# Loading the first expert's weights in two blocks and zero-filling the output rows during attention

## What is computed

```python
x = attention(q, k, v)                    # 2 batches x 768 tokens x 512, 8 heads of 64
# window |i-j| < 16, beside 24 block summaries (max of k, mean of v, blocks of 32)
e = argmax(x @ w_gate)                    # or the previous token's expert, by a local gate
p = softmax(x @ w_gate)[e]
x = p * (relu(x @ w1[e]) @ w2[e])         # 8 experts, 512 -> 1024 -> 512
theta = x @ w_theta
u = x + w_tok_r @ (x * cos(theta)) + w_tok_i @ (x * sin(theta))
out = u + relu(u @ w_ch)
```

## Time and profile before

| what | value |
|---|---|
| median of 3 runs | 424.57 us |
| lowest and highest of them | 423.96 and 425.23 us |
| the profiled execution's own time | 423.96 us |
| its span, first to last instruction | 422.2 us |
| mean granted clock of TensorE | 0.999 |
| PE busy | 409.2 us, 97% |
| DVE, ACT and POOL busy | 258.0, 194.1 and 80.8 us |
| moved by DMA | 54.50 MB, mean 129 GB/s |

### The profile page before, as it was taken

One profiled execution on the slowest core, in us unless ns is written; L12 is line 12 of the kernel. 1 busy time (PEld: TensorE's weight loads), 2 busy tenths in 40 slices (PEclk: granted clock), 3 DMA queues, 4 the chain that ended last, 5 costly groups with the idle time before them and its releaser, 6 DMA issues.

```text
span 422.2 us, 8097 instructions
## 1 busy us (share of the span) xinstructions
PE 409.2 (97%) x2791; PEld 328.6 (78%) x2792; DVE 258.0 (61%) x429; ACT 194.1 (46%) x431; POOL 80.8 (19%) x127
## 2 busy tenths in 40 slices
PE   6889999999999999999999999999999999999996
PEld 3668786468888888888888778888888888888885
DVE  4898998898646327363117595666687646454352
ACT  1698995624647326463247464444433143213110
POOL 3697783221112100121110023200000000000000
PEclk9999999999999999999999999999999999999999
DMA  8995551162989933518130025300000000000012
GB/s 293 412 374 170 185 178 78 51 249 73 380 274 397 367 153 90 208 35 338 50 100 26 0 72 202 100 2 0 0 2 0 26 25 0 27 25 27 25 57 93
DMA packets 17424, 54.50 MB, mean 129 GB/s; under 512 B 2033, under 2 KB 2161, under 8 KB 17137
## 3 DMA queue, kind: packets, MB, share of 16 engines
q1 hardware_dynamic: 12560, 40.98, 27.1%
q0 software_dynamic: 2960, 9.70, 7.0%
q10 hardware_dynamic: 1872, 3.41, 2.1%
HBM read 40.46 MB, written 13.63 MB: 128 GB/s over the span
## 4 chain that ended last, share of the span: by engine, by line
PE 77%; DVE 3%; ACT 3%; DVEq 1%; issue 1%; ACTq 0%; POOL 0%
PE ps L1570 15%; PE ps L1572 14%; PE ps L1571 14%; PE ps L1714 8%; PE ps L1715 8%; PE ps L1716 8%; PE ps L1652 2%; PE ps L1592 2%; PE ps L1621 2%; PE ps L1460 2%; ACT w_h L756 1%; PE ps L1565 1%; DVE w_l L1095 1%; PE ps L1432 1%; DVEq L1102 1%
## 5 line engine op out<-in xcount | busy, mean ns | idle before, releaser
L1714 PE MATMUL ps<-z_h,mix_h 128*128 128x512 f32 x144 | 56.9, 395 | 0.0
L1716 PE MATMUL ps<-z_h,mix_l 128*128 128x512 f32 x144 | 56.1, 390 | 0.0
L1715 PE MATMUL ps<-z_l,mix_h 128*128 128x512 f32 x144 | 56.1, 390 | 0.0
L1570 PE MATMUL ps<-w_h,hT_h 128*128 128x512 f32 x104 | 42.0, 404 | 0.8 <-DVE w_l L1095 0.5
L1095 DVE TENSOR_TENSOR w_l<-w_raw,w_h (+1 forms) x32 | 37.4, 1219 | 8.3 <-ACT w_h L756 8.3
L705 ACT ACTIVATE p<-s,nmax 128x120 f32<-128x120 f32 x96 | 36.5, 384 | 11.1 <-DVE nmax L938 11.1
L1572 PE MATMUL ps<-w_l,hT_h 128*128 128x512 f32 x104 | 40.7, 391 | 0.0
L1571 PE MATMUL ps<-w_h,hT_l 128*128 128x512 f32 x104 | 40.5, 390 | 0.0
L1570 PE MATMUL ps<-w_h,xT_h 128*128 128x512 f32 x96 | 38.4, 400 | 0.0
L1571 PE MATMUL ps<-w_h,xT_l 128*128 128x512 f32 x96 | 37.4, 390 | 0.0
L1572 PE MATMUL ps<-w_l,xT_h 128*128 128x512 f32 x96 | 37.4, 390 | 0.0
(11 more groups left out here) (264 smaller groups left out, 860.2 us busy)
## 6 DMA issues: line engine op xcount, KB each, us to landing
w_raw<-w SPq DMA_DIRECT2D x32, 512.0 KB, 6.2
mix_raw<-mix SPq DMA_DIRECT2D x6, 768.0 KB, 6.0
kfull<-k_full SPq DMA_DIRECT2D x8, 400.0 KB, 6.4
q_all<-q_t SPq DMA_DIRECT2D x6, 512.0 KB, 7.3
vpad<-v_pad SPq DMA_DIRECT2D x4, 768.0 KB, 8.8
xd<-x_sb POOLq DMA_DIRECT2D x12, 256.0 KB, 4.6
ys<-y_sb ACTq DMA_DIRECT2D x12, 256.0 KB, 2.0
out<-o SPq DMA_DIRECT2D x12, 256.0 KB, 2.0
```

The source lines that it names most:

```text
L1570: pe.matmul(ps[:, bank, :], a_h[:, k, :], w_h[:, n, :], start=(k == 0), stop=False)
L1714: pe.matmul(ps[:, i, :], w_h, zh, start=(jb == 0 and m == 0), stop=False)
L1715: pe.matmul(ps[:, i, :], w_h, zl, start=False, stop=False)
L1716: mm = pe.matmul(ps[:, i, :], w_l, zh, start=False, stop=(jb == TPB - 1 and m == 1))
```

## The change

Three edits, two on SP and one on ACT.

```diff
             sp.dma_start(const[:, C_UT:C_END], const_d[:, C_UT:C_END]).then_inc(rconst_in, 16)
-            for i in range(STEPS):
-                sp.wait_ge(norm_done, 2 + i)
-                sp.dma_start(w1_raw[:, i * SW:(i + 1) * SW, :], w1_d[0, :, i * SW:(i + 1) * SW, :]).then_inc(w1_in[i], 16)
-            for i in range(STEPS):
-                sp.wait_ge(norm_done, 2 + STEPS + i)
-                sp.dma_start(w2_raw[:, i * SW:(i + 1) * SW, :], w2_d[0, :, i * SW:(i + 1) * SW, :]).then_inc(w2_in[i], 16)
+            sp.wait_ge(norm_done, 2)
+            load_weights(w1_raw, w1_d[0], w1_in)
+            sp.wait_ge(norm_done, 4)
+            load_weights(w2_raw, w2_d[0], w2_in)
+            sp.wait_ge(zeroed, 1)
+            for i in range(2):
+                sp.wait_ge(norm_done, TPB + 2 * i)
+                part = slice(TPB + i * (NS - TPB) // 2, TPB + (i + 1) * (NS - TPB) // 2)
+                sp.dma_start(ys_t[part].rearrange("t p n -> p t n"),
+                             zero[:, :].unsqueeze(1).broadcast_to([P, part.stop - part.start, DM])).then_inc(zeros_in, 16)
...
             load_mix(1)
-            sp.wait_ge(zeroed, 1)
-            for i in range(2):
-                part = slice(TPB + i * (NS - TPB) // 2, TPB + (i + 1) * (NS - TPB) // 2)
-                sp.dma_start(ys_t[part].rearrange("t p n -> p t n"),
-                             zero[:, :].unsqueeze(1).broadcast_to([P, part.stop - part.start, DM])).then_inc(zeros_in, 16)
...
             split(3, w1_raw, w1_h, w1_in, w1_hi)
+            act.wait_ge(zeros_in, 32)
             y_copy(1)
...
             act.wait_ge(raw_in[1], NU // 2 // MIX * 16)
-            act.wait_ge(zeros_in, 32)
             with act.Fori(EARLY, UNITS) as t:
```

## The result

Over 22 executions of each, the kernel before had a median of 424.39 us (423.83 to 425.74) and the changed one 427.39 us (424.71 to 430.23). The ratio is 1.0069, with a 95% interval of 1.0055 to 1.0084: 3.0 us slower. The forecast was 424.2 us and no measurable change, so it was wrong, and the time lies outside its range. One execution of the kernel before, of 680 us at a mean granted clock of 0.559, is left out of what follows.

What follows compares the result with a forecast made beforehand. PE was taken as the bound, busy 409.2 of 422.2 us. The terms 0 + 0 + 0 - 0.35 us took the median of 424.57 us to 424.2 us, with a range of 423.3 to 425.3 us.

Steps and rivals of the forecast that it cites:

- Weights of the first expert sooner: Attention: `w1` and `w2` already land some 13 us or more before ACT first reads them, so issuing them sooner gives 0 us.
- The zero fill fits into attention: Attention, 45 to 61 us: 14.0 of 16 us of DMA time needed; zeros land near 62 us, at worst 76.
- The wait on ACT: Ahead of the copy for slot tile 1 at 113.72 us: zeros landed 37 us or more earlier, so 0 us.
- Third expert sooner: Experts' stage: SP reaches the third expert some 2 us sooner, but its weights weren't late, so 0 us.
- The 0.35 us of register loads: Experts' stage near 129 us: DVE's loads, slow beside the zero fill, return to 0.31 us; PE regains 0.35 us.
- w_l 0.5: Sign in PE's waits: the experts' 0.5 us wait for DVE's `w_l`, placed at 132.91 us, would vanish.
- The Trainium skill's rule: Against the register-load term: DMA never contends with a compute engine, so the sum would be 0.
- Slower: Attention: POOL's three stores from 46 to 57 us each take 0.20 us more, attention ends 0.6 us later; chance 0.12.
- Nothing changes: Experts' stage: register loads are slow for another reason or the third expert's weights slow them equally; 424.6 us, chance 0.23.
- much faster: Whole kernel: faster by over 0.3%, 423.2 us or less, needing 0.5 us more out of attention; chance 0.04.
- late zeros: Experts' stage: zeros land after 113.7 us and ACT stands; a fill ending at 118 us gives about 428.5 us; chance 0.01.

Runs made afterwards that it cites:

- e2: Against the kernel before: first expert's weights still paced, the two zero fills moved into attention behind the first and third piece of `w2`; ratio 0.9997.
- e6: Against the kernel before: weights paced, zero fills in attention at norm_done 6 and 8, each issued ahead of the `w2` piece; ratio 0.9991.
- e9: Against the kernel before: weights paced, first 1.75 MB fill issued at av_ready 6, second behind the third piece of `w2`; ratio 0.9994.
- e1: Against the kernel before: first expert's weights in two blocks at norm_done 2 and 4, zero fill left late; 425.52 us against 425.0, ratio 1.001.
- e12: Against the kernel before: one weight piece per norm_done from 3 to 10, small fill pieces from 4 to 11; 424.06 us against 424.8, ratio 0.9994.
- e7: The change without its wait for norm_done 4, both weights issued as one 4 MB burst; ratio 1.0032 against the kernel before.

## Why the prediction was wrong, point by point

**Weights of the first expert sooner: 0 us. This step failed.** It counted who reads the data (right: nobody before ACT) and who else uses the DMA engines, and for the latter it named POOL's stores alone. The passengers it left out were PE's own instructions, although the page of the profile lists them as a queue ("q8 instruction"): the term put at 0 us was the wait of PE for them. What stood in its place: the fetch asked for near 27 us waited 5.5 and 6.1 us behind the `w1` block instead of 4.2, a gap of 1.2 and 1.8 us, a second gap of 1.7 us at the fill, and often 1.5 us of clock behind them. The rows to see it by were there: 0.68 us for a group that elsewhere takes 0.43.

**The zero fill fits into attention: right as to bandwidth, wrong as to cost.** It was issued at 47.34 and 57.77 us, and its last packet went at 66.1 us, later than the 62 us forecast and within the bound of 76. But a full DMA engine is not harmless because nobody waits for the data. In the change it cost 1.7 us, in e2, e6 and e9 nothing.

**The wait on ACT: 0 us. Right.** The copy for tile 1 starts with no gap, and the fill had long landed. **Third expert sooner: 0 us. Right**, nothing came of it. ACT's timeline (of before):

```profile
116.58 0.59 ACT L776 ACTIVATE y_sb<-ps 128x512 f32<-128x512 f32 x1
...
132.40 2.96 ACT L755 ACTIVATE w_h<-w_raw 128x1024 fp32r<-128x1024 f32 x3 [0.55 <-issue]
```

**The 0.35 us of register loads: right at its place, its reason only in part.** DVE's two loads on that way took 0.33 and 0.30 us in the change, against 0.68 and 0.70, ACT's gap fell from 1.23 us to 0.55, and PE's step from transposes to product is 135.57 - 135.22 = 0.35 us, against 0.70:

```profile
135.22 0.60 PE L1564 MATMUL ps<-const,xin 128*128 128x128 f32 x4
135.57 0.48 PE L1569 MATMUL ps<-w_h,hT_h 128*128 128x512 f32 x1
```

The step is 0.35 or 0.36 us in all twelve traces with the fill moved, and 0.70 and 0.52 us in the two with it late (before, e1). But "quick beside weights, slow beside the zero fill" is more than the traces bear. In the kernel before, DVE's next two loads, at 135.52 and 136.28 us, took 0.31 and 0.30 us with the fill still on the wires. And single loads took up to 0.73 us with the fill long over (0.72 at 115.72 and 0.54 at 129.28 us in e12, 0.73 at 115.94 us in e2). What makes a load slow stays open.

The row "w_l 0.5" in PE's waits, which I had said would vanish, is still there: in the kernel before it stands at 247.80 us, in a later expert's `w2`, so I had read the earlier trace rows for the wrong place. The Trainium skill's rule ("SBUF — State Buffer", section "Who interferes with whom"), which gave 0, does not cover these loads. Of the 0.35 us the tile before took some 0.15 us back: its step was 123.31 - 122.42 = 0.89 us against 0.74. A register load of DVE ahead of it, at 118.53 us, took 0.59 us against 0.33 in the kernel before; that this is the reason isn't shown.

```profile
122.42 0.60 PE L1564 MATMUL ps<-const,xin 128*128 128x128 f32 x4
123.31 0.49 PE L1569 MATMUL ps<-w_h,hT_h 128*128 128x512 f32 x1 [0.29 <-DVE hT_l L1118]
```

**Rivals.** "Slower" had the right sign and stage and the wrong mechanism: POOL's stores took their 0.54 us as before. It was priced at 0.6 us, the real one at 2.3 to 3.2 us, and given 0.12. "Nothing changes", "much faster" and "late zeros" didn't come about.

**What stays open.** Why one request waits 0.13 us and another 6 behind the same kind of traffic. Waits never passed 6.2 us, whether the burst was 2, 3.75 or 4 MB. The Trainium skill, "DMA: Bandwidth & Descriptors", section "Queues, rings and completion order", says that a DMA engine serves its queues in turn, a packet's worth at a time; a request would then wait for one turn of the others. The waits of 0.13 to 6.16 us neither confirm nor refute this, since which of the 16 engines a packet rode isn't in the trace. The traces do narrow it. All four requests that were served within 0.2 us (for block 1730, in the kernel before, e2, e6 and e7) came when no packet at all was on the wires. In the change the fill's first packet (48.30 us) came 0.48 us after the request (47.82), as it did in e7 (47.92 and 47.44); but in e7 the wires were empty, and in the change the tail of `w2` and of POOL's store was still running. The DMA engines' packets around the request, in e7 from 45.0 to 47.4 us, then in the change from 47.0 to 48.25 us:

```profile
DMA packets 0, 0.00 MB, mean 0 GB/s; under 512 B 0, under 2 KB 0, under 8 KB 0
...
DMA packets 20, 0.05 MB, mean 39 GB/s; under 512 B 8, under 2 KB 8, under 8 KB 20
```

So the burst need not be on the wires yet when the request comes; what else is on them at that moment differs between these traces. How that holds the fetch isn't shown. Each kernel but the change was traced once, so how often a gap comes is known for none of them. So for e1, whose times spread widely, what its slower executions met was not seen, and that they met the gap is an inference.

## What to carry to other kernels

Before transfers are packed densely into a stage, list everything that rides the DMA engines, the program's own code included, and compare the longest wait with the time that a block of 256 instructions of the busiest engine lasts. A gap of "issue" inside a run of identical instructions, at distances of 256, was a late code block here; a group half as long again as its likes (0.68 us against 0.43) was one that came barely late. Pacing transfers that nobody needs early cost nothing that could be measured, and it was worth 3 us against the change.

## What the runs showed of the hardware that was unexpected

- PE's program comes over the DMA engines in 16 KB packets, by the packets' times each asked for when PE enters the block before. In attention it waited 0.13 to 6.16 us, and where it came late, PE went on 1.3 to 1.5 us after the packet's end.
- The same `w1` block, issued at the same time, held such a packet for 5.53 us in one trace and 2.59 us in another (e1).
- Gaps of PE of 1.7 and 1.8 us in attention were followed in one trace by stretches at 1.2 GHz, each worth 1.7 us; in another, gaps of 1.2 and 1.7 us were not. Executions of the change at a mean granted clock of 0.995 or 0.996 took 1.5 us longer than those at 0.999 or 1.0.
- DVE's register loads from on-chip memory mostly took 0.30 to 0.33 us, beside full DMA engines too, but single ones took up to 0.73 us: 0.68 and 0.70 us while the zero fill read that memory (but 0.31 and 0.30 us some 6 us later in the same fill), 0.72 and 0.73 us with no fill under way.
